# Attention, mixture, routed mixture: the sixth pass of the dense mixture in block form, with the routing of the last two token groups moved into and behind its second layer

## The reference

```python
x = attention(q, k, v)          # 2 x 8 heads x 768 x 64, window of 16 plus pooled blocks of 32
x = x.transpose(0, 2, 1, 3).reshape(1536, 512)

# dense mixture: 4 experts, all of them for every token
p = domain_probs / (domain_probs.sum(-1, keepdims=True) + 1e-09)
for e in range(4):
    h = np.maximum(x @ w1[e], 0.0)               # 512 -> 1024
    out += p[:, e:e + 1] * (h @ w2[e])           # 1024 -> 512

# routed mixture: 8 experts, one for each token that has x @ w_skip > 0
logits = xc @ w_gate
e_idx = np.argmax(logits, axis=1)
gate_w = probs[np.arange(len(xc)), e_idx]
for e in range(8):
    h = np.maximum(xc[mask] @ v1[e], 0.0)        # mask: e_idx == e
    y[mask] = gate_w[mask, None] * (h @ v2[e])
out[do_compute] = xc + y                         # the other tokens keep x
```

## Time and profile before

| | us |
|---|---|
| median of 3 runs | 736.73 (736.33 to 738.81) |
| the profiled execution | 737.65 |
| its span, first to last instruction | 735.9 |
| TensorE busy | 708.9 |
| VectorE busy | 402.9 |
| ScalarE busy | 277.6 |

### The profile page before, as it was taken

The page is one execution under the profiler, slowest core; times in us unless marked ns, Lnnn a source line. Parts: engine busy times, 40 slices in busy tenths (PEclk is TensorE's granted clock), DMA queues, the critical chain, the costliest instruction groups (busy, mean ns, idle before and its releaser), DMA issues.

```text
span 735.9 us, 12370 instructions
## 1 busy us (share of the span) xinstructions
PE 708.9 (96%) x4530; PEld 585.1 (80%) x4531; DVE 402.9 (55%) x1039; ACT 277.6 (38%) x637; POOL 66.3 (9%) x97
## 2 busy tenths in 40 slices
PE   5599999999999999999999999999999999999997
PEld 5488898888988879988988997898898985444444
DVE  4977674452886483782756364366542255544341
ACT  4645454451345433631621451056031202542430
POOL 2611000000000000000000000100100012333221
PEclk9989999999999999999999999999999999999999
DMA  9874632111618707623076729123224279599900
GB/s 205 221 194 108 142 71 63 34 45 41 246 56 344 309 7 265 286 79 114 1 298 273 266 106 381 46 90 115 86 86 172 86 291 352 207 398 395 385 6 21
DMA packets 90672, 126.77 MB, mean 172 GB/s; under 512 B 55000, under 2 KB 55276, under 8 KB 89200
## 3 DMA queue, kind: packets, MB, share of 16 engines
q1 hardware_dynamic: 87952, 121.30, 48.4%
q0 software_dynamic: 2656, 4.66, 1.9%
HBM read 98.81 MB, written 27.64 MB: 172 GB/s over the span
## 4 chain that ended last, share of the span: by engine, by line
PE 76%; DVE 10%; DMA 9%; issue 2%; SPq 1%; ACT 1%; POOL 0%; DVEq 0%; POOLq 0%
PE ps L1782 14%; PE ps L1784 14%; PE ps L1783 14%; PE ps L2047 5%; PE ps L2049 5%; PE ps L2048 5%; PE ps L2197 4%; PE ps L2169 4%; DMA w_aside<-wb_lo 3%; DMA sets<-in_moe_w 3%; PE ps L1844 2%; PE ps L1816 2%; PE ps L1990 1%; PE ps L1830 1%; DVE wb_lo L1368 1%
## 5 line engine op out<-in xcount | busy, mean ns | idle before, releaser
L2047 PE MATMUL ps<-xt_hi,wb_hi 128*128 128x384 f32 x280 | 94.2, 337 | 1.7 <-ACT h_raw L981 1.4
L2049 PE MATMUL ps<-xt_hi,wb_lo 128*128 128x384 f32 x280 | 93.7, 335 | 0.0
L2048 PE MATMUL ps<-xt_lo,wb_hi 128*128 128x384 f32 x280 | 93.7, 335 | 0.0
L981 ACT ACTIVATE h_raw<-ps 128x384 f32<-128x384 f32 x80 | 39.1, 490 | 93.1 <-PE ps L2049 91.3
L1783 PE MATMUL ps<-v_lo_acc,hb_hi 128*128 128x512 f32 x180 | 70.2, 390 | 0.0
L1782 PE MATMUL ps<-xt_hi,w_hi 128*128 128x384 f32 x184 | 64.2, 349 | 0.3 <-DVE h_lo L1224 0.3
L1784 PE MATMUL ps<-xt_hi,w_lo 128*128 128x384 f32 x184 | 61.8, 336 | 0.0
L1783 PE MATMUL ps<-xt_lo,w_hi 128*128 128x384 f32 x184 | 61.7, 335 | 0.0
L1382 DVE TENSOR_TENSOR h_raw<-ps,h_raw 128x384 f32<-128x384 f32 x80 | 41.4, 553 | 37.0 <-PE ps L2049 36.9
L916 ACT ACTIVATE h_hi<-ps 128x384 fp32r<-128x384 f32 x48 | 23.6, 491 | 94.7 <-PE ps L1784 69.4
L1397 DVE SCALAR_TENSOR_TENSOR acc<-ps,dp,acc 128x512 f32<-128x512 f32 x30 | 22.5, 750 | 66.0 <-PE ps L1784 66.0
(11 more groups left out here) (268 smaller groups left out, 1343.6 us busy)
## 6 DMA issues: line engine op xcount, KB each, us to landing
sets<-in_moe_w SPq DMA_DIRECT2D x72, 512.0 KB, 7.4
acc<-in_moe_w SPq DMA_DIRECT2D x10, 768.0 KB, 5.2
w_aside<-wb_hi SPq DMA_DIRECT2D x2, 3584.0 KB, 16.6
w_aside<-wb_lo SPq DMA_DIRECT2D x2, 3584.0 KB, 24.8
wb_hi<-w_aside SPq DMA_DIRECT2D x14, 512.0 KB, 11.9
wb_lo<-w_aside SPq DMA_DIRECT2D x14, 512.0 KB, 12.7
w_raw<-in_moe_w SPq DMA_DIRECT2D x12, 512.0 KB, 5.5
stage<-in_moe_w SPq DMA_DIRECT2D x8, 512.0 KB, 4.4
```

The source lines that it names most:

```text
L981: nc.scalar.activation(h_raw[:, f, half * GT:(half + 1) * GT], ps[:, bank, 0:GT], ACT.Copy).then_inc(put_by, 1)
L2047: mm(to, wb_hi[w], hi(c), start=(c == 0 and not onto), stop=False, skip_group_check=onto)
L2048: mm(to, wb_hi[w], lo(c), start=False, stop=False, skip_group_check=onto)
L2049: last = mm(to, wb_lo[w], hi(c), start=False, stop=(c == HALF_D - 1), skip_group_check=onto)
```

## The change

`PASSES` is no longer cut: there are six passes, `LAST` = 5 is expert 3 on half 1, and `KEPT` becomes 3, so that the blocks of all three experts are saved and read back. The raw load, the splitting and both plain groups behind the passes are gone. The routing of groups 2 and 3 goes into layer 2 of pass 5 and behind it. The turned tiles of these groups and the rows and inputs of the first tiles lie in a new piece of memory (`under`) over the block weights. The list of the two first tiles is closed with group 1 (`HALVES` in place of `G - 1`), so their rows are gathered when layer 1 of pass 5 ends. SyncE loads the sets from there on. Two smaller edits: the block sums of the next pass move one tile later on VectorE, and pass 0 gets the late places of the second weights that pass 3 had, which are themselves shifted by one part.

```diff
-    PASSES = [(b, e) for b in range(B) for e in range(1, E1)][:-1]
+    PASSES = [(b, e) for b in range(B) for e in range(1, E1)]
...
-            if t == SWITCH:
-                return ((), (), (), (), (), (0,), (1, 2), (3, 4), (5, 6, 7))[2 * i + slot]
+            if t in (0, SWITCH):
+                return ((), (), (), (), (), (0, 1), (2, 3), (4, 5), (6, 7))[2 * i + slot]
...
+                if t <= SWITCH:
+                    sp.wait_ge(blocks_saved, 32 * t)
...
             gp.wait_ge(first_ids_ok, 1)
             for k in range(STARS):
-                gather_rows(k, ids(k), GT * (G - 1))
+                gather_rows(k, ids(k), GT * HALVES)
             send_entries(G - 2)
+            gp.wait_ge(x1_kept, 16 * (G - 1))
             gp.wait_ge(x1_rest, 16)
+            gp.wait_ge(rows_done, TPH * len(PASSES))
             gp.wait_ge(first_ids_ok, 2)
             gather_rows(STARS, ids(STARS))
...
                 if t + 1 < SWITCH:
-                    if tt == 0:
+                    if tt == 1:
                         block_sums(t + 1, 0)
                         block_sums(t + 1, 1)
-                    if tt == 1:
+                    if tt == 2:
                         low_blocks(t + 1, range(3))
-                    if tt == 2:
+                    if tt == 3:
                         low_blocks(t + 1, range(3, BLOCKS))
...
+                if t == LAST and tt == 4:
+                    copy_x(0, 0)
+                    choose(G - 2)
...
+                        if t == LAST and tt == TPH - 1 and k == FP:
+                            route_logits(GR * (G - 1))
+                            route_turn(GR * (G - 1) + 1)
...
+                    if t == LAST:
+                        if tt == 1:
+                            route_turn(TPH)
+                        if 2 <= tt <= 4:
+                            route_logits(TPH + tt - 2)
+                            route_turn(TPH + tt - 1)
+                        if tt == 3:
+                            first_rows(0, 0)
...
+            route_rank(G - 2)
             route_logits(last_row - 1)
-            first_rows(0)
-            route_turn(last_row)
             pe.wait_ge(set_in[0][0], 16 * PIECES)
             step = layer1_steps(1, 0)
             next(step)
+            route_turn(last_row)
+            next(step)
             route_logits(last_row)
             next(step)
+            list_first(G - 2)
             next(step)
+            first_rows(1, bank_x(1))
             route_rank(G - 1)
-            next(step)
-            list_first(G - 1)
-            pe.wait_ge(sum_ok, G)
-            mm(ps[:, 3, 0:E2], ones[:, :], hot_sum[:, G, :], start=True, stop=True).then_inc(count_ps, 1)
-            first_rows(1)
             turn_h(1)
-            layer1(2, 0)
+            for j, _ in enumerate(layer1_steps(2, 0)):
+                if j == 0:
+                    list_first(G - 1)
```

More of the change, by code:

```diff
@@ L2080, in factors, with transpose_x, first_rows @@
                     block(t, S3, i, sum_of(T3), BX, True)
+            def transpose_x(rows, bank=4):
+                for j in range(DQ // P):
+                    last = nc.tensor.transpose(ps[:, bank, j * P:(j + 1) * P], rows[:, j * P:(j + 1) * P], ident[:, :])
+                last.then_inc(x_tr, 1)
+            def first_rows(k, bank):
+                pe.wait_ge(gathered[k], 16)
+                transpose_x(xg[k], bank)
             def rows_out(t, fill):
```

253 lines of the change are left out of this document (80 added, 173 removed).

## The result

The changed kernel takes **728.43 us** (median of 4 runs, 727.93 to 730.36), the kernel before beside it 736.53 us (4 runs, 736.24 to 738.81). The ratio is 0.9889, with a 95% interval from 0.9866 to 0.9912: faster by 8.1 us, and outside the 0.3% that can be told from no change. 728.2 was forecast. The profiled execution was the slowest of the four: 730.36 us, with a span of 728.6; the three others had spans of 726.2 to 726.9. Three executions in a later batch took far longer than the rest (789.63 and 796.42 us of two kernels, 2467.27 us of the kernel before); medians and ratios leave them out.

The account below looks back on a forecast made before the run. TensorE was taken to bound most of the kernel, and a chain from group 3's routing through gather and set loads the tail. 4.2 + 5.8 - 1.5 = 8.5 us less gave a median of 728.2 us, range 725.8 to 732.6.

Parts of the forecast that it names:

- Part 1, early stalls: Passes 0 to 3: four TensorE waits vanish through the two small order edits, worth 4.2 us (bounds 0 to 4.2).
- The first rival: Passes 0 to 3: the early stalls stay in another form, since the transfers do not move; 732.4 us, chance 0.11.
- Part 2, block form: Pass 5: block form with routing inside replaces the plain form, 68.0 us for 73.8, so 5.8 us less.
- E: The point where the last matmul of the sixth layer 2 is issued: forecast at 601.5, before at 611.52.
- Part 3, the routing of group 3: Behind E: entries of group 3 come 1.5 us later against E (bounds 0.5 and 3); nothing changes behind them.
- The doubt on the DMA: Third tile's gather: 6.3 us if it meets SyncE's backlog, some 2.5 if engines take turns; the forecast took 6.3.
- That the tail gains more: Tail: emptier queues, third gather 2.5 us, TensorE waits for nothing until the fourth tile; 726.3 us, chance 0.10.
- Sets that come late for the first tile: First tile's second layer waits for its set, a stall of 13 us at 240 GB/s; 741 us, chance 0.04.
- A sixth tile of the star: Star's rows: three padded rows more make a fifteenth tile in all; 736.4 us, chance 0.03.
- used up waiting for gather and list: Second tile: TensorE reaches it at E + 8.0, before 8.6; the spare time goes to waiting.
- seventh tile near 653.7, still behind a set load: Sign in the tail: the seventh tile starts near 653.7, waiting for a set load, with 14 tiles as now.
- the seventh tile waits for nothing: Sign of failure in the tail: if the seventh tile has no wait, the forecast's mechanism is wrong.

Follow-up runs that it names:

- changed_again: The changed kernel itself, unedited, run once more in another batch: 729.33 us, ratio 0.9893 to the kernel before.
- pieces_ahead: Changed kernel with layer 2 of expert 2's set (2 MB) issued behind the star's eighth piece, ahead of the fourth set: 731.34 us, ratio 0.9916.
- set_no_wait: Changed kernel with layer 2 of the fourth set no longer held back until the fourth tile's gather has landed: 733.2 us, ratio 0.9939.
- sets_behind: Changed kernel with layer 2 of expert 2's set (2 MB) issued behind the rows of group 3, not ahead of them: 731.38 us, ratio 0.9924.
- copy_first: Changed kernel with VectorE's copy of the fourth tile's rows ahead of gates and addition, two register reads ahead of the list wait: 728.97 us, ratio 0.989.
- copy_and_busy: Changed kernel with the fourth tile's rows copied ahead of gates and addition, plus 12 spare transposes ahead of that tile's gathered rows: 729.20 us, ratio 0.9887.

## Why the prediction was right, and where it was not

**Part 1, early stalls (4.2 us): right.** Pass 1 starts at 276.50 (forecast 276.5), pass 5 4.2 us earlier, and the edits alone give 4.3 us (by its interval 3.4 to 5.3). The step from start to start was the right measure: the modelled waits add up to 3.6. The first rival, that the stalls take another form, is out.

**Part 2, block form (5.8 us): right.** From the start of pass 5 to E it takes 601.32 - 533.48 = 67.8 us, forecast 68.0. Layer 1 has 168 matmuls in 29.15 us, layer 2 takes 38.7 (39), with no wait at a turn or a logit. E stands at 601.32, forecast 601.5.

**Part 3, the routing of group 3 (1.5 us later against E): the entries 0.3 us short, and the chain behind them not as it was.** The first list stands at E + 9.3 (8.8), the entries end at E + 12.2 (about 12; 613.56 for 613.4), which is 1.8 us later than before and not 1.5. So the term of 1.5 us was sized 0.3 us too small. The forecast let nothing change behind the entries, and that step does not hold: from the entries to the issue of the fourth tile's gather it was 631.84 - 621.96 = 9.9 us and is now 624.03 - 613.56 = 10.5. All of this 0.6 is in two transfers: the last scatter takes 2.54 us where it took 2.11, the reading of the list 2.63 where it took 2.43. In `changed_again` it is 10.3, and there the set loads give 0.5 back (27.25 us to the seventh tile for 27.75). E to the seventh tile is then 52.4 us, after 50.65: 1.8 us lost, near the forecast's 1.5 because a loss and a gain that it did not have cancel.

**The doubt on the DMA: taken the wrong way, and it cost nothing.** I took 6.3 us for the third gather, by the row of before. It took at most 3.6, and TensorE did not wait for it. It does meet the last of the backlog, as forecast: issued at E + 11.2, with the DMA full until about E + 13.6. The step that failed is the price: the 6.3 us of before belong to about 4.6 us of full engines behind the issue, and here there were about 2.4. It cost nothing in the sum since the tail hangs on the fourth tile's gather. The Trainium skill ("DMA: Bandwidth & Descriptors", section "Queues, rings and completion order") says that an engine changes between queue rows after each packet; by this a gather on GpSimd's queue need not wait for SyncE's backlog. The trace of `pieces_ahead` agrees so far, that the gather landed some 2.3 us ahead of the end of the backlog. But this does not give the forecast's "some 2.5 us": under load it took 5.65 us there and 7.56 in `set_no_wait`, 3 to 5 us more than with idle engines. What exactly slows it, the packets of the loads between its own or the memory, these runs do not tell apart.

**The rivals.** That the tail gains more (726.3) did not come, though TensorE waited for nothing until the fourth tile, as that rival has it: the chain to the seventh tile does not begin there. Sets that come late for the first tile showed in neither profiled execution of the changed kernel; in `sets_behind` they did, a stall of 2.6 us for 2 MB more ahead of the eighth piece, though the end moved by the late scatter and not by the stall. The tiles stayed 14, with 73.7 us from the seventh to the end in both kernels. (A sixth tile of the star would have taken four padded rows more, not three: 317 + 3 rows still fill five tiles of 64.)

**What was not foreseen.** The pause at the fourth tile, 1.4 us for its gather and 1.4 us for VectorE's copy. The forecast spoke only of spare time "used up waiting for gather and list". The pause costs nothing while the clock holds, since the seventh tile waits for its set anyway; removing it moved the wait (`copy_first`). With it the granted clock fell to 0.50 in one of the two profiled executions of this kernel, worth 1.5 us at the fourth tile and, after the set's slack, about 1 us at the seventh (28.23 for 27.25). The statement "seventh tile near 653.7, still behind a set load" is therefore true of the second of them (653.54, 0.5 us of waiting) and not of the first (654.89, none). By the forecast's own sign ("the seventh tile waits for nothing") the mechanism fails in the first, and the lower clock is the reason. Execution for execution: 729.15 was forecast for the profiled one; the second has 729.00, the first 730.36.

**Luck.** The median of 728.43 lies 0.2 us from the forecast, closer than the kernel repeats itself: the other batch has 729.33, at ratio 0.9893 for 0.9889. The sum had no term for the clock, which fell in one profiled execution of two.

## What to carry to other kernels

Price a change in the chain that sets the end, and find where that chain begins: here what was done for TensorE and VectorE at the fourth tile came back as a wait at the seventh, 27 us behind the start of the set loads, while of the 10.2 us saved ahead of E 8.1 came through. A stall that shows on TensorE need not be what a change costs: in two kernels the loss went by a scatter that took 2 us longer under load. Small edits to the order in which a worker asks for data and empties results were worth as much (4.3 us) as removing 24 matmuls and a routing block (3.7). Issue a small gather that others wait for ahead of the bulk loads, or hold these back until it has landed, as the wait of SyncE does here: without it the kernel lost 3.4 to 3.7 us.

## What the runs showed of the hardware

- An indirect gather of one tile took at most 2.6 us with little else in flight (DMA share 0.07 from 624.0 to 626.6), 5.65 us at a share of 1.06 (`pieces_ahead`), and 7.56 us behind 2 MB of loads issued 1.2 us ahead of it on another engine's queue, with more issued behind it (`set_no_wait`). In `pieces_ahead` it landed while that backlog had some 2.3 us to run.
- The last scatter of the list took 2.1 to 2.5 us with the DMA nearly idle (before, changed), and 4.5 to 4.7 us beside full loads (`pieces_ahead`, `sets_behind`).
- After two waits with six transposes between them the granted clock fell to 0.50 in three profiled executions (1.4 and 1.4 us in the changed kernel, 1.9 and 1.4, 1.2 and 1.4) and stayed at 1.00 in two (1.3 and 1.4 in the same kernel, 0.8 and 1.4); after a single wait of 1.9 us it fell in `copy_first` and stayed in `copy_and_busy`. Where it fell, 16 matmuls took 4.99 to 5.35 us in place of 3.65. With 12 or 24 spare transposes in the pause it stayed at 1.00 at the fourth tile in all three kernels that have them, one profiled execution each.
- The core's DMA moved 398 GB/s over 23 us at a share of 1.04 in the changed kernel, and 398 GB/s from 640 to 662 us in the kernel before.
